# Up-projections as Strassen's seven block products, with weight sums kept in DRAM

## What is computed

```python
sig = 1.0 / (1.0 + np.exp(-f_logit))
f = lower_bound + (1.0 - lower_bound) * sig
h[t] = f[t] * h[t-1] + (1 - f[t]) * x[t]          # per token t, per feature
a = h @ w_in0;  g = a * (1.0 / (1.0 + np.exp(-1.702 * a)));  x1 = g @ w_out0
b = x1 @ w_in1; g = np.where(b >= 1, b, np.where(b <= -1, 0.0, (b + 1) ** 2 / 4)); out = g @ w_out1
```

## Time and profile before

| | before |
|---|---|
| device time, median of 3 | 1097.5 us |
| profiled execution, span from first to last instruction | 1095.3 us |
| PE busy | 1067.3 us, 97% |
| VectorE, ScalarE, GpSimd busy | 54%, 49%, 51% |
| first matmul | 21.3 us |
| DMA traffic | 27.5 MB, 25 GB/s on average |

### The profile page before, as it was taken

One profiled execution on the slowest core, in us unless ns is written; L12 is line 12 of the kernel. 1 busy time (PEld: TensorE's weight loads), 2 busy tenths in 40 slices (PEclk: granted clock), 3 DMA queues, 4 the chain that ended last, 5 costly groups with the idle time before them and its releaser, 6 DMA issues.

```text
span 1095.3 us, 13955 instructions
## 1 busy us (share of the span) xinstructions
PE 1067.3 (97%) x4632; PEld 867.7 (79%) x4632; DVE 591.5 (54%) x825; ACT 541.4 (49%) x899; POOL 563.5 (51%) x416
## 2 busy tenths in 40 slices
PE   2999999999999999999999999999999999999998
PEld 2778888888888888888888888888888888888887
DVE  7758556446445555644645554554464464433553
ACT  4565554445445445445544544544544454454443
POOL 2676555544544554554554454455455455444443
PEclk9999999999999999999999999999999999999999
DMA  4322000100100100100010010010001000000000
GB/s 166 123 96 71 7 1 20 39 1 19 38 0 19 38 0 0 38 19 0 19 38 0 19 38 0 19 38 0 0 19 38 0 19 0 0 20 1 1 20 17
DMA packets 8181, 27.46 MB, mean 25 GB/s; under 512 B 993, under 2 KB 1761, under 8 KB 8161
## 3 DMA queue, kind: packets, MB, share of 16 engines
q1 hardware_dynamic: 8160, 27.20, 6.7%
HBM read 20.97 MB, written 6.23 MB: 25 GB/s over the span
## 4 chain that ended last, share of the span: by engine, by line
PE 93%; DVE 3%; ACT 1%; issue 1%; POOL 0%; DMA 0%; SPq 0%; POOLq 0%; DVEq 0%
PE hid L253 47%; PE acc L253 47%; DVE act_g L446 1%; ACT g_hi L368 1%; DVE gate L463 1%; DVE state L493 1%; ACT act_t L363 0%; DVE in0lo L190 0%; DMA lb<-lower_bound_dram 0%; DVE gate L470 0%; POOL g_lo L568 0%; SPq L225 0%; POOL in_chunk1lo L190 0%; DVE drive L477 0%; POOLq L95 0%
## 5 line engine op out<-in xcount | busy, mean ns | idle before, releaser
L568 POOL TENSOR_TENSOR g_lo<-act_g,g_hi 128x512 fp32r<-128x512 f32 (+1 forms) x384 | 521.1, 1357 | 512.9 <-ACT g_hi L368 512.9
L368 ACT ACTIVATE g_hi<-act_g 128x512 fp32r<-128x512 f32 (+1 forms) x384 | 241.3, 628 | 304.7 <-DVE act_g L446 156.9
L446 DVE SCALAR_TENSOR_TENSOR act_g<-act_t,hid 128x512 f32<-128x512 f32 (+1 forms) x192 | 130.4, 679 | 191.9 <-ACT act_t L363 168.1
L438 DVE TENSOR_SCALAR act_t<-hid 128x512 f32<-128x512 f32 (+1 forms) x192 | 131.8, 686 | 139.0 <-PE hid L253 138.8
L450 DVE SCALAR_TENSOR_TENSOR act_g<-hid,act_t 128x512 f32<-128x512 f32 (+1 forms) x192 | 131.7, 686 | 132.8 <-ACT act_t L366 122.5
L366 ACT ACTIVATE act_t<-act_t 128x512 f32<-128x512 f32 (+1 forms) x192 | 120.6, 628 | 137.0 <-DVE act_t L438 136.8
L253 PE MATMUL hid<-in0hi,w_up0hi 128*128 128x512 f32 (+2 forms) x360 | 141.7, 394 | 21.3 <-DVE in0lo L190 21.3
L363 ACT ACTIVATE act_t<-hid 128x512 f32<-128x512 f32 (+1 forms) x192 | 113.2, 589 | 92.1 <-PE hid L253 91.2
L253 PE MATMUL acc<-g_hi,w_down0hi 128*128 128x512 f32 (+1 forms) x384 | 152.3, 397 | 1.4 <-POOL g_lo L568 1.4
L253 PE MATMUL acc<-g_hi,w_down1hi 128*128 128x512 f32 (+1 forms) x384 | 152.3, 397 | 0.2 <-POOL g_lo L568 0.2
L253 PE MATMUL acc<-g_hi,w_down0lo 128*128 128x512 f32 (+1 forms) x384 | 150.5, 392 | 0.0
(11 more groups left out here) (56 smaller groups left out, 1060.2 us busy)
## 6 DMA issues: line engine op xcount, KB each, us to landing
drive<-x_dram SPq DMA_DIRECT2D x12, 512.0 KB, 4.2
gate<-f_logit_dram SPq DMA_DIRECT2D x11, 512.0 KB, 3.3
out_dram<-staging SPq DMA_DIRECT2D x11, 512.0 KB, 2.6
staging<-w_in_dram SPq DMA_DIRECT2D x8, 512.0 KB, 3.7
staging<-w_out_dram SPq DMA_DIRECT2D x8, 512.0 KB, 3.5
gate<-f_logit_dram SPq DMA_DIRECT2D x2, 256.0 KB, 3.2
out_dram<-staging SPq DMA_DIRECT2D x1, 448.0 KB, 3.0
lb<-lower_bound_dram SPq DMA_DIRECT2D x1, 1.0 KB, 3.6
```

The costliest lines, as they stand in the source:

```text
L368: act.activation(g_hi[:, s % RING, 0:n], g, ACT.Copy).then_inc(s_ghi, 1)
L438: dve.tensor_scalar(t, hidden, -1.0, 1.0, ALU.max, ALU.min).then_inc(s_clip, 1)
L446: dve.scalar_tensor_tensor(out=g, in0=t, scalar=1.0, in1=hidden, op0=ALU.add, op1=ALU.mult).then_inc(s_g, 1)
L568: pool.tensor_tensor(g_lo[:, s % RING, 0:n], act_g[:, s % RING2, 0:n], g_hi[:, s % RING, 0:n].bitcast(F32), ALU.subtract).then_inc(s_glo, 1)
```

## The change

Tokens are cut into seven chunks of two halves of n tokens, n = 384, 384, 512, 512, 512, 512, 224. A stage is again one layer of one chunk, but has 8 groups, each of two blocks of 128 hidden units. In a group the up-projection is a 2x2 block product (weights: two feature blocks by two hidden blocks; inputs: two feature blocks by two token halves). It is computed in Strassen's manner (Winograd's form) from seven products of 128x128 weights with 128xn inputs, each three matmuls as before, instead of eight. The seven weight operands are four blocks and sums of them (`A..`, `S..`), the seven inputs are blocks and sums (`B..`, `T..`). The results, four tiles C11, C22, C12, C21 of 128xn hidden values, share partial sums: three products accumulate in one bank, `chain`, whose states after the first, second and third product are copied out by ACT (`take`, to `snap` in SBUF); DVE adds a snapshot to another bank and writes the tile to SBUF (`evac`, to `hid`) for C11, C22 and C21, while C12 is read from `chain`. The down-projection (`unit`) is unchanged in arithmetic: 24 matmuls a group. The order on PE alternates products of group G with units of group G - 1.

The split weight operands of a group (14 tiles of 128x128, 896 KB in fp32r) no longer fit for all groups. They are made during the stages in which a layer is first used (stage 0 for layer 0, stage 2 for layer 1): DVE forms four sums (`up_sums`), ACT the high part (`up_hi`), DVE the low part (`up_lo`); SP writes them to `up_scratch` in DRAM, and in all other groups reads them back into one of two buffers (`load_up`). The inputs need three sum instructions (`x_sum`), seven high copies (`x_hi`) and four low instructions (`x_lo`) for each stage, in fixed places 0, 1, 2 of DVE's group. The down weights are made in the same groups (`down_hi` on ACT, `down_lo` on POOL). The loops over chunks are written out.

The diff, cut to its core (waits on SP for the first groups, the start and the host's reordering of the arrays are left out):

```diff
+HALF = (384, 384, 512, 512, 512, 512, 224)
+CHUNKS = len(HALF)
+BASE = [4 * P * sum(HALF[:c]) for c in range(CHUNKS + 1)]
+assert 2 * sum(HALF) == TOKENS
...
+STAGES = [(0, 0), (0, 1)]
+for _c in range(2, CHUNKS):
+    STAGES += [(1, _c - 2), (0, _c)]
+STAGES += [(1, CHUNKS - 2), (1, CHUNKS - 1)]
...
+A11, A12, A22, S1, S2, S3, S4 = range(7)
+B11, B21, B22, T1, T3, T2, T4 = range(7)
+P1, P2, P6, P7, P5, P3, P4 = range(7)
+W_OF = {P1: A11, P2: A12, P6: S2, P7: S3, P5: S1, P3: S4, P4: A22}
+X_OF = {P1: B11, P2: B21, P6: T2, P7: T3, P5: T1, P3: B22, P4: T4}
+C11, C22, C12, C21 = range(4)
+F_OF = (0, 1, 0, 1)
...
+            def save_up(G):
+                l, g = STAGES[G // NG][0], G % NG
+                if G == 0:
+                    sp.wait_ge(s_wup0, 1)
+                else:
+                    sp.wait_ge(s_wup, made_n(G) - 1)
+                sp.dma_start(scratch[l * NG + g], w_up[G % RING][:].rearrange("p a j f -> p (a j f)").bitcast(F32))\
+                  .then_inc(s_saved[g], 16)
...
+            def load_up(G):
+                l, g = STAGES[G // NG][0], G % NG
+                sp.wait_ge(s_prod, product_n(G - RING, P4))
+                if is_made(G - RING):
+                    sp.wait_ge(s_saved[(G - RING) % NG], 16 * (STAGES[(G - RING) // NG][0] + 1))
+                sp.wait_ge(s_saved[g], 16 * (l + 1))
+                sp.dma_start(w_up[G % RING][:].rearrange("p a j f -> p (a j f)").bitcast(F32), scratch[l * NG + g])\
+                  .then_inc(s_loaded[G % RING], 16)
...
+            for G in range(GROUPS):
+                si, g = divmod(G, NG)
+                if is_made(G + 1) and G >= 0:
+                    save_up(G + 1)
+                if is_made(G + 2):
+                    load_raw_up(G + 2)
+                    load_raw_down(G + 2)
+                if G + 2 < GROUPS and not is_made(G + 2):
+                    load_up(G + 2)
+                if g == 0 and si > 0 and STAGES[si - 1][0] == 1:
+                    store(si - 1)
+                if si % 2 == 0 and si + 1 in SCANNED and g == (7 if si == 0 else 6):
+                    sp.wait_ge(s_xlo, low_n(si + 1, 3))
+                    load_chunk(SCANNED[si + 1])
...
+            def product(G, j, bank, start):
+                n = half(G // NG)
+                b = (G // NG) % 2
+                w, xs = W_OF[j], X_OF[j]
+                three(bank[:, 0:n], [w_up[G % RING][:, part, w, :] for part in range(2)],
+                      [xin[b][part][:, xs, 0:n] for part in range(2)], start, True, not start).then_inc(s_prod, 1)
+            def unit(G, u):
+                si, g = divmod(G, NG)
+                l, n = STAGES[si][0], half(si)
+                i, d = divmod(u, K)
+                t, s = T_OF[i], 2 * g + F_OF[i]
+                start, stop = g == 0 and i in (C11, C22), g == NG - 1 and i in (C12, C21)
+                if is_made(G) and u == 0:
+                    pe.wait_ge(s_wdown, made_n(G))
+                if start and si > 0:
+                    pe.wait_ge(s_z[d], 2 * (si - 1) + (1 if t == 1 else 2))
+                sums = acc[d][t][:, 0:n]
+                w = [w_down[l][part][:, s, d * P:(d + 1) * P] for part in range(2)]
+                if d == 0:
+                    pe.wait_ge(s_ghi, tile_n(G, i))
+                pe.matmul(sums, w[0], g_hi[i][:, 0:n], start=start, stop=False)
+                if d == 0:
+                    pe.wait_ge(s_glo, tile_n(G, i))
+                pe.matmul(sums, w[0], g_lo[i][:, 0:n], start=False, stop=False)
+                pe.matmul(sums, w[1], g_hi[i][:, 0:n], start=False, stop=stop).then_inc(s_unit, 1)
+            for G in range(GROUPS):
+                si, g = divmod(G, NG)
+                if G == 0:
+                    pe.wait_ge(s_wup0, 1)
+                elif is_made(G):
+                    pe.wait_ge(s_wup, made_n(G) - 1)
+                else:
+                    pe.wait_ge(s_loaded[G % RING], 16 * (loads_before(G) + 1))
+                if g == 0 and si == 0:
+                    pe.wait_ge(s_xlo_pair, 1)
+                elif g == 0:
+                    pe.wait_ge(s_xlo, low_n(si, 3))
+                if G >= 2:
+                    pe.wait_ge(s_g, tile_n(G - 2, C12))
+                product(G, P1, chain[G % 2], True)
+                if G >= 1:
+                    unit(G - 1, 0)
+                    pe.wait_ge(s_evac, third_n(G - 1, 0))
+                product(G, P2, single, True)
+                if G >= 1:
+                    unit(G - 1, 1)
+                if G == 0:
+                    pe.wait_ge(s_xlo_first, 1)
+                pe.wait_ge(s_snap, third_n(G, 0))
+                product(G, P6, chain[G % 2], False)
+                if G >= 1:
+                    unit(G - 1, 2)
+                    pe.wait_ge(s_evac, third_n(G - 1, 2))
+                if G == 0:
+                    pe.wait_ge(s_xlo_first, 2)
+                product(G, P7, pair, True)
+                if G >= 1:
+                    unit(G - 1, 3)
+                pe.wait_ge(s_snap, third_n(G, 1))
+                product(G, P5, chain[G % 2], False)
+                if G >= 1:
+                    unit(G - 1, 4)
+                    unit(G - 1, 5)
+                if G == 0:
+                    pe.wait_ge(s_xlo_first, 3)
+                pe.wait_ge(s_snap, third_n(G, 2))
+                product(G, P3, chain[G % 2], False)
+                if G >= 1:
+                    unit(G - 1, 6)
+                if G == 0:
+                    pe.wait_ge(s_xlo_first, 4)
+                pe.wait_ge(s_evac, third_n(G, 1))
+                product(G, P4, pair, False)
+                if G >= 1:
...
+            def take(G, k):
+                n = half(G // NG)
+                act.wait_ge(s_prod, product_n(G, (P1, P6, P5)[k]))
+                if G >= 1:
+                    act.wait_ge(s_evac, third_n(G - 1, (0, 2, 1)[k]))
+                act.activation(snap[k][:, 0:n], chain[G % 2][:, 0:n], ACT.Copy).then_inc(s_snap, 1)
...
+                c = SCANNED.get(si)
+                if c is not None and g < 4:
+                    exp_step(c, g)
+                if is_made(NG * si + g + 1):
+                    up_hi(NG * si + g + 1)
...
+            def x_lo(si, k):
+                n = half(si)
+                first, tiles, many = ((B11, source_of(si), 2), (B22, source_of(si), 1), (T1, sums_of(si), 2),
...
+                hi, lo = (xin[si % 2][part][:, first:first + many, 0:n] for part in range(2))
+                dve.tensor_tensor(lo, view, hi.bitcast(F32), ALU.subtract).then_inc(s_xlo, 1)
...
+            def up_sums(G):
+                k = 4 * (made_n(G) - 2)
+                dve.wait_ge(s_raw_up, 16 * made_n(G))
+                dve.tensor_tensor(raw_up[:, 4, :], raw_up[:, 0, :], raw_up[:, 3, :], ALU.add).then_inc(s_wsum, 1)
+                dve.tensor_tensor(raw_up[:, 6, :], raw_up[:, 1, :], raw_up[:, 0, :], ALU.subtract).then_inc(s_wsum, 1)
+                dve.wait_ge(s_wsum, k + 1)
+                dve.tensor_tensor(raw_up[:, 5, :], raw_up[:, 4, :], raw_up[:, 1, :], ALU.subtract).then_inc(s_wsum, 1)
+                dve.wait_ge(s_wsum, k + 3)
+                dve.tensor_tensor(raw_up[:, 7, :], raw_up[:, 2, :], raw_up[:, 5, :], ALU.subtract).then_inc(s_wsum, 1)
+            def up_lo(G):
+                dve.wait_ge(s_wup_hi, made_n(G))
+                dve.tensor_tensor(w_up[G % RING][:, 1], raw_up[:, 1:8, :], w_up[G % RING][:, 0].bitcast(F32),
+                                  ALU.subtract).then_inc(s_wup, 1)
...
+            def evac(G, k):
+                n = half(G // NG)
+                i = (C11, C22, C21)[k]
+                bank = (single, pair, pair)[k]
+                dve.wait_ge(s_prod, product_n(G, (P2, P7, P4)[k]))
+                dve.wait_ge(s_snap, third_n(G, (0, 2, 1)[k]))
+                dve.tensor_tensor(hid[i][:, 0:n], bank[:, 0:n], snap[(0, 2, 1)[k]][:, 0:n], ALU.add).then_inc(s_evac, 1)
+            def clip(G, i):
+                n = half(G // NG)
+                if i == C12:
+                    dve.wait_ge(s_prod, product_n(G, P3))
+                    hidden = chain[G % 2]
+                else:
+                    dve.wait_ge(s_evac, third_n(G, {C11: 0, C22: 1, C21: 2}[i]))
+                    hidden = hid[i]
+                dve.wait_ge(s_glo, tile_n(G - 1, i))
+                dve.tensor_scalar(g_act[i][:, 0:n], hidden[:, 0:n], -1.0, 1.0, ALU.max, ALU.min).then_inc(s_clip, 1)
...
+            def recurrence(c, a, place):
+                np = len(pieces(HALF[c]))
+                if place == 1:
+                    for r in (2 * (a - 1), 2 * (a - 1) + 1):
+                        if 0 <= r < 4 * np:
+                            reciprocal_step(c, r // np, r % np)
+                for q in range(4):
+                    at = 1 + (np * (q + 1) - 1) // 2
+                    if place == 2 and a == at:
+                        f_step(c, q)
+                    if place == 0 and a == at + 1:
+                        drive_step(c, q)
```

(96 more changed lines are left out.)

873 lines of the change are left out of this document (476 added, 397 removed).

## The result

The changed kernel takes 1232.9 us (median of 4 runs, 1231.6 to 1235.7) where the kernel before, beside it, took 1096.1: a ratio of 1.1245, interval 1.1222 to 1.1269. It is slower, as forecast, but by 137 us where 52 were forecast, and it lies above the range of 1105 to 1185.

A forecast was written before the change was run, and what follows sets the result against it. PE, busy 1067.3 of 1095.3 us, was taken to bound the kernel. Its matmuls fall to 1002, with start and end 1039, and stalls and weight making add 110: 1149 us, range 1105 to 1185 (8 in 10: 1058 to 1190).

The forecast's parts named there:

- PE's work: All matmuls: 45 a group where 48 were, 1002 us in all, 67 less than 1069.5.
- The exclusion: DVE instructions on SBUF (two inputs or fast mode) and POOL's subtractions exclude each other; a bare layer-1 group takes 10.75, not 10.45.
- the side engines fit: Rival: added stalls give slack elsewhere; only start, half of making and a few seams remain, 1064 us; chance 0.32.
- Bare groups, n = 512: Layer-1 groups of 512 columns without extras: clip C21 blocked by POOL's subtraction makes them 10.75 us against PE's 10.5.
- Layer 0, n = 512: Stages 88 us each, four 350 against 336; input work ahead of evac C11 stalls groups 3 and 5 by 1.2 and 1.8.
- Making the weights: Stage 0: groups 1 to 3 12 us each, seven groups 74 against 55.6; stage 2: 88 against 63.5.
- the sign it named: Stage 0: DVE over 90% busy would show the forecast.
- the start: Twelve reciprocals, sums and low parts come first; group 0 ends at 37.5 us, against 7.9 of matmuls.
- Stage 1: Recurrence of a 512-wide chunk beneath 384-wide groups: 69 us against 63.5.
- Short stages: Two stages of 224 columns: 90 us against 76, groups of 5.6 in layer 1 and 5.4 in layer 0.
- Weights arrive late: Rival: late weight loads or something unseen in the seams add 24 to 50 us, 1185; chance 0.05.
- The clock: Rival: starved PE falls to 1.2 GHz in stages 0 and 2, 35 us more, 1184; chance 0.05.

The follow-up runs named there:

- e1: Changed kernel with GpSimd's g_lo subtraction cut to 64 columns in all but two groups, so low parts are mostly stale; 1145.1 us, 88 less.
- e9: Changed kernel with ACT doing up_hi, exp and inc ahead of the activation of C11 in making groups but a stage's first; 1217.6 us, 15 less.
- e5: Changed kernel with up_lo moved from place 1 to place 2 of DVE's group; 1253.6 us, 21 more.
- e4: Changed kernel with the read-back of weight operands cut to 512 of 7168 bytes a partition, the rest stale; 1226.1 us, 7 less.
- e6: Changed kernel with x_lo of layer-0 stages moved from place 0 to 1 and x_sum one place back in layer-1 stages; 1194.9 us, 38 less.
- e12: Changed kernel with six chunks, tiles summed in PSUM, input work and up_hi reordered, weight sums on GpSimd, reciprocals spread; 1094.3 us, ratio 0.9985 to the kernel before.
- e7: Changed kernel with halves of 480, 512, 512, 512, 512, 512 instead of seven chunks; 1195.9 us, ratio 1.0911 to the kernel before, 37 less.

## Why the prediction was right in direction and short in size

- **PE's work**: right. Twelve starts of 384 columns have a pitch of 0.175 (predicted 0.177), twelve of 224 one of 0.112 (predicted 0.105, with 0.120 as bound), so the work of the two short stages is 81 us where 76 stood in the sum.
- **The exclusion**: right in mechanism and phase, and the rival *the side engines fit* fell. It was short in size: the forecast priced it in one crossing a group (10.75 for 10.45), 1.5 us of `x_lo` in a layer-1 stage and 2 us in each of the first three made groups, to name the largest; by e1 88 us hang on it. The Trainium skill (SBUF — State Buffer, section "SBUF: two separate sides") has the rule, and by e1 the trace agrees.
- **Bare groups, n = 512**: 10.76 measured for 10.75, and by PE's first matmuls layer 1 as a whole is right to 4 us in 360. (DVE's eleven tile instructions, summed as 6.8, come to 7.1 at the forecast's own prices; nothing hung on it.)
- **Layer 0, n = 512**: 88 to 91 by the takes for 88, which looks better than it is. Groups 3 take 12.9 to 14.0 for 11.7 and groups 5 12.1 to 13.7 for 12.3, and the shorter first groups of this reading hide it; by PE's first matmuls it is 362 for 350. In e1 both stalls are gone: they were the order of input work, as forecast, but together with the blocking, which the forecast left out there.
- **The step that failed**: "Making the weights". Its 12 us for groups 1 to 3 of stage 0 measured 14.3, its 38.2 for groups 4 to 7 46.8, and the same sum for stage 2, 88, measured 102.4. It added up DVE's busy time and an allowance for blocking and took DVE to be the limit; the sign it named, DVE over 90% busy in stage 0, did not come (73%). The real group has 11.3 us busy and 3.0 of waits for ACT inside DVE's queue, which e9 shortened and e5 lengthened. With the start (first take of group 1 at 42.2 for 37.5) it makes 20 us in stage 0 and 14 in stage 2.
- **Stage 1, 69 for 80**: an instruction was overlooked. Its last group already makes stage 2's first weights and takes 13.2 us. In its seam ACT waits 2.8 us for the load of `f_logit` (e4 takes 2.8 off the seam).
- **Short stages, 97 for 112**: in stage 11 the second group takes 11.5, because `x_sum` waits 5.1 us for the store of `zout`. The forecast looked at this store only as something in front of a load. Its groups 3 to 5 take 6.7, 6.8 and 6.4 for 5.4, which is the order of input work: in e6 they take 5.4, 5.5 and 5.2. In stage 13 the middle groups take 6.1 to 6.3 where 5.6 was walked, and 5.8 or 5.9 in e1, so half of that excess or more is blocking.
- **Weights arrive late** was true in no place where PE stood: a load of 896 KB landed in 4.5 us (median) where 5 to 6.5 were reckoned. What the weights' traffic delayed was another load and a store, for 7 us by e4.
- **The clock** fell, which no row of before showed, and it began low. The record of the granted clock starts at 44.7 us, and the 33 matmuls in front of it stand 0.32 apart and not 0.175:

```profile
42.84 0.52 PE L272 MATMUL single<-xin0hi,w_up 128*128 128x384 f32 x1
43.16 0.52 PE L272 MATMUL single<-xin0lo,w_up 128*128 128x384 f32 x1
```

That is 4.8 us at most (1.7 for the 18 slow ones of the kernel before), which the mean clock of 0.93 in stage 0 leaves out. Behind 44.7 the mean of 0.979 over the run makes 2 x 0.021 x 1230 = 52 us at the lower level, 1.2 GHz. 140 matmuls start in it; at the pitches of either level (0.320 for 0.175 with 384 columns, 0.427 for 0.233 with 512, 0.213 for 0.112 with 224) they cost some 20 us more, an estimate from above, since in the making groups PE had time to spare. The Trainium skill (TensorE: Matmul & The Clock Gate, "Part 1") says that the clock falls when the engine idles, and the trace agrees: each fall stands behind a gap of PE (below), and in e12, which has no gap over 1.6 us from 51 us on, none stands between there and the end. As a rival of its own (1184) it was priced too high in its place, but not at all in the forecast. How much of the 20 us reached the end was not separated from the gaps.

## What to carry to other kernels

When work moves from an engine that was full to engines that were half empty, busy sums do not price it: walk the in-order queue of the helper through one whole period, with every wait for the third engine in its place, and look for a ring. Put in the waits for buffers that a DMA still reads or fills, too: here a store held up a sum for 5 us. Before giving VectorE tiles in SBUF beside a GpSimd that works all the time, see whether the tile can be summed in place in PSUM (42 us here), and whether the small SBUF-only work fits GpSimd itself (9.6 us in stage 0 alone; 22 in all, with the reciprocals spread). Choose the chunks so that none is so narrow that hand-offs outlast its matmuls (37 us in e7).
